# Routed experts: the first slot's expert chosen from the first 16 tiles, its weights loaded under the last dense group, and the gates gathered from memory

## The reference, cut to what matters

```python
def _moe2_ref(x, expert_emb, tau, w1, w2):        # N, D, E, F = 3072, 384, 8, 1024
    xn = x / (norm(x) + 1e-06)
    en = expert_emb / (norm(expert_emb) + 1e-06)
    logits = xn @ en.T / tau
    expert_idx = np.argmax(logits, axis=1)
    probs = np.exp(logits - logits.max(-1, keepdims=True))
    probs /= probs.sum(-1, keepdims=True) + 1e-09
    gate_w = probs[np.arange(N), expert_idx]
    for e in range(E):
        mask = expert_idx == e
        h = np.maximum(x[mask] @ w1[e], 0.0)
        out[mask] = gate_w[mask, None] * (h @ w2[e])
...
def reference(**kwargs):
    attn_out = _attn_ref(**attn_kwargs)            # B, H, S, D = 4, 8, 768, 48: delta rule
    x = attn_out.transpose(0, 2, 1, 3).reshape(B * S, H * D)
    x = _moe_ref(x=x, **moe_kwargs)                # all 8 experts on all rows, Sinkhorn gates
    return _moe2_ref(x=x, **moe2_kwargs)           # each row to its best expert
```

## Time and profile before

| | us |
|---|---|
| median of three runs | 2285.17 (2283.51 to 2286.48) |
| the profiled execution's own time | 2289.73 |
| its span, first to last instruction | 2287.9 |
| TensorE busy | 2201.0 (96%) |
| DVE busy | 1013.8 (44%) |
| ACT busy | 600.7 (26%) |
| POOL busy | 96.5 (4%) |

### The profile page before, as it was taken

One profiled execution on the slowest core, in us unless ns is written; L12 is line 12 of the kernel. 1 busy time (PEld: TensorE's weight loads), 2 busy tenths in 40 slices (PEclk: granted clock), 3 DMA queues, 4 the chain that ended last, 5 costly groups with the idle time before them and its releaser, 6 DMA issues.

```text
span 2287.9 us, 42621 instructions
## 1 busy us (share of the span) xinstructions
PE 2201.0 (96%) x17911; PEld 2041.4 (89%) x17911; DVE 1013.8 (44%) x1888; ACT 600.7 (26%) x1019; POOL 96.5 (4%) x91
## 2 busy tenths in 40 slices
PE   4899999999999999999999999999999998799998
PEld 4888899999999998999999899999999998699998
DVE  7676556245333333333233332323333235767774
ACT  2323222331111111111111111111111122366664
POOL 0000000000000000000000000000000000122221
PEclk7799999999999999999999999999999999699999
DMA  9545543340000000000000000000000011667662
GB/s 315 158 136 140 145 127 109 87 159 28 1 28 1 29 28 1 28 1 28 1 28 28 1 28 1 28 1 28 1 1 1 1 42 42 210 241 249 231 234 73
DMA packets 152504, 172.69 MB, mean 75 GB/s; under 512 B 81580, under 2 KB 112464, under 8 KB 152338
## 3 DMA queue, kind: packets, MB, share of 16 engines
q1 hardware_dynamic: 143090, 158.70, 21.6%
q0 software_dynamic: 3968, 10.82, 1.2%
q10 hardware_dynamic: 5280, 0.66, 0.2%
HBM read 144.19 MB, written 27.33 MB: 75 GB/s over the span
## 4 chain that ended last, share of the span: by engine, by line
PE 88%; DVE 5%; DMA 2%; SPq 2%; issue 2%; ACT 1%; POOL 0%; POOLq 0%; ACTq 0%; DVEq 0%
PE psA L1703 22%; PE psH L1720 16%; PE psB L1703 9%; PE psB L1720 8%; PE psY L1720 8%; PE psY L1845 6%; PE psH L1597 4%; PE psY L1612 3%; PE psB L1831 3%; PE psA L1831 3%; PE psA L1478 3%; DVE products L1046 1%; DVE sx L1049 1%; DMA r_scratch<-sr 1%; SPq L405 1%
## 5 line engine op out<-in xcount | busy, mean ns | idle before, releaser
L1703 PE MATMUL psA<-X,wh 128*128 128x512 f32 x1440 | 449.4, 393 | 1.8 <-DVE acc L1068 0.9
L1214 DVE SCALAR_TENSOR_TENSOR hl<-psA,hh 128x512 fp32r<-128x512 f32 x240 | 165.7, 690 | 626.6 <-ACT hh L846 626.5
L846 ACT ACTIVATE hh<-psA 128x512 fp32r<-128x512 f32 x240 | 143.3, 597 | 830.3 <-PE psA L1703 830.3
L1703 PEld LDWEIGHTS psA<-X,wh 128*128 128x128 f32 x1440 | 265.9, 188 | 47.5 <-issue 3.4
L1703 PE MATMUL psA<-X,wl 128*128 128x512 f32 x720 | 284.9, 396 | 0.0
L1720 PE MATMUL psH<-wh,hh 128*128 128x384 f32 x672 | 228.3, 340 | 0.0
L1720 PE MATMUL psH<-wh,hl 128*128 128x384 f32 x672 | 227.2, 338 | 0.0
L1720 PE MATMUL psH<-wl,hh 128*128 128x384 f32 x672 | 225.8, 336 | 0.0
L1214 DVE SCALAR_TENSOR_TENSOR hl<-psB,hh 128x512 fp32r<-128x512 f32 x96 | 66.3, 691 | 277.4 <-ACT hh L846 277.3
L1703 PE MATMUL psB<-X,wh 128*128 128x512 f32 x576 | 179.2, 392 | 0.0
L1438 DVE TENSOR_TENSOR vl<-vs,vh 128x768 fp32r<-128x768 f32 x152 | 145.6, 961 | 56.6 <-ACT vh L891 56.2
(11 more groups left out here) (282 smaller groups left out, 4122.9 us busy)
## 6 DMA issues: line engine op xcount, KB each, us to landing
vs<-v_d SPq DMA_DIRECT2D x38, 768.0 KB, 6.0
vs<-v_d SPq DMA_DIRECT2D x19, 1536.0 KB, 11.8
ws<-w_d SPq DMA_DIRECT2D x28, 768.0 KB, 6.0
kT<-kT_d SPq DMA_DIRECT2D x17, 512.0 KB, 5.3
qT<-qT_d SPq DMA_DIRECT2D x15, 512.0 KB, 5.3
a_scratch<-an SPq DMA_DIRECT2D x12, 512.0 KB, 4.0
kq<-kn_d SPq DMA_DIRECT2D x6, 768.0 KB, 6.2
vn<-vn_d SPq DMA_DIRECT2D x12, 384.0 KB, 4.9
```

What stands on the lines that cost most here:

```text
L846: act.activation(hh[kk % 3][:, :], ps_h[kk % (2 if last else 3)], ACT.Relu).then_inc(hh_ready, 1)
L1214: dve.scalar_tensor_tensor(hl[b][:, :], ps_h[bank], 0.0, hh[b][:, :].bitcast(F32), ALU.max, ALU.subtract).then_inc(hl_ready, 1)
L1703: mm = pe.matmul(to, a[half][:, c, col], X[:, 2 * g:2 * g + 2, b, c, :], start=(n == 0), stop=(n == 3 * KC - 1))
```

## The change

What it does, part by part:

1. `choose(0)`, `prefixes(0)`, `ranks(0)` and `places(0)` run one step earlier in the last expert, `counts(0)` on TensorE too. `places` 4 and 8 stand before `choose(1)`.
2. `most_rows` (five small DVE instructions) finds the expert with the most rows in tiles 0 to 15, `star`. `order_of_big` (five more) makes an order of experts in which it comes first, and `grown` uses it for the big slots; three instructions correct `eid` for it.
3. SP loads that expert's weights after the stores of the first ten chunks (groups 0 to 4), as soon as `star_i` and the first half's weight buffers are free. The buffers of the dense weights are laid out anew, so that slot 0's `vs` lie over the first half's, and the routing's small tensors over the dense hidden activations. Slot 1's weights now also wait for slot 0's rows (`xg_in[0]`).
4. ACT splits slot 0's eight pieces ahead of `features(0)`. DVE splits four ahead of it, two behind it and the last two in blocks 0 and 1 of slot 0. Slot 1's eight pieces are split two a block in blocks 4 to 7 of slot 0.
5. The gates' table, `entry_g` and its 24 products are gone. The norms and the exponential stand in blocks 1 and 2 of slot 0, the reciprocal in block 3. TensorE transposes the gates in block 4, DVE copies them, SP stores them to `g_dram` (two DMAs), and POOL gathers them by `who` for each slot (31 indirect DMAs of 128 values). ACT waits for them (`gates_in`) before it scales. TensorE's `features(1)` waits for DVE's copy.
6. `who` is written before the last instructions of `eid`.

```diff
-FIRST = 2
+FIRST = 4
+FIRST_LATE = 6
+GATED = 2
+SECOND_SPLIT = {4: (0, 1), 5: (2, 3), 6: (4, 5), 7: (6, 7)}
...
+                    if c == 2 * (NTA // GT + 1):
+                        sp.wait_ge(star_ready, 1)
+                        sp.wait_ge(l2_done, STEPS * (E - 2) + STEPS // 2)
+                        load_weights(sp.value_load(star_i[0:1, 0:1], min_val=0, max_val=E - 1), 0)
                     sp.wait_ge(acc_done, NALL - NT + GT * (c // 2 + 1))
...
                 sp.wait_ge(eid_ready, 1)
-                load_weights(0, 0)
-                load_weights(1, 1)
+                sp.wait_ge(xg_in[0], 16 * ST)
+                load_weights(expert_of(1), 1)
+                sp.wait_ge(gate_ready, 1)
+                for g in range(2):
+                    rows = g_dram[2 * g * S:2 * (g + 1) * S, :].rearrange("(t k) o -> t (k o)", k=C)
+                    sp.dma_start(rows, gate_rows[:, g * C:(g + 1) * C]).then_inc(gate_out, 16)
...
+                def gather_gates(i):
+                    for s in range(1 if SMALL[i] else ST):
+                        u = COLUMN[i] + s
+                        pool.indirect_dma_start(gates[:, u:u + 1], None, g_dram,
+                                                bass.IndirectOffsetOnAxis(who[:, u:u + 1], 0)).then_inc(gates_in[i % 2], 16)
...
                 gather(0)
                 gather(1)
+                pool.wait_ge(gate_out, 32)
+                gather_gates(0)
+                gather_gates(1)
                 for i in range(2, NSLOT):
                     gather(i)
                     scatter(i - 2)
+                    gather_gates(i)
...
-                        if last and kk == STEPS - 3:
+                        if last and kk == STEPS - 4:
                             choose(0)
-                        if last and kk == STEPS - 2:
+                        if last and kk == STEPS - 3:
                             prefixes(0)
-                        if last and kk == STEPS - 1:
+                        if last and kk == STEPS - 2:
+                            most_rows()
                             ranks(0)
+                        if last and kk == STEPS - 1:
+                            places(0)
+                            order_of_big()
...
-                        if next_small is not None:
+                        if not reached(i, 1):
+                            if f + FIRST_LATE < KF:
+                                split_piece(0, 0, f + FIRST_LATE)
+                            if f == GATED - 1:
+                                gate_norms()
+                            if f == GATED + 1:
+                                gate_values()
+                            if f == GATED + 2:
+                                gate_copy()
+                            for q in SECOND_SPLIT.get(f, ()):
+                                split_piece(1, 1, q)
+                        elif next_small is not None:
                             split_piece(i + 1, 1 - par, f)
...
-                    if kk == STEPS - 2:
+                    if kk == STEPS - 3:
                         counts(0)
...
+                        if f == GATED + 2 and not reached(i, 1):
+                            pe.wait_ge(gate_made, 1)
+                            pe.transpose(ps_gate, gate[:, :, :].rearrange("p b c -> p (b c)"), ident).then_inc(gate_turned, 1)
                         if f == 5 and after:
+                            if not reached(i, 1):
+                                pe.wait_ge(gate_ready, 1)
                             features(i + 1, 1 - par, *after)
...
                 features(0, 0, False, ST)
-                table(entry_g, entry_g_ready, ps_tab[1]).then_inc(tab_g_done, 1)
```

More of the change, by code:

```diff
@@ L160, in build @@
         w_at = top[0]
[L161 to L165, removed]
+        half_w = 4 * KC * FH
+        assert half_w == 4 * FB * DM
+        wh1, wh2, wl1, wl2 = [], [], [], []
+        for i in range(2):
+            wh1.append(keep(f"wh1_{i}", [P, KC, FH], F32R))
+            wh2.append(keep(f"wh2_{i}", [P, FB, DM], F32R))
+            wl1.append(keep(f"wl1_{i}", [P, KC, FH], F32R))
+            wl2.append(keep(f"wl2_{i}", [P, FB, DM], F32R))
         h_at = top[0]
@@ L175, in build @@
         kq = [keep(f"kq{i}", [P, 2 * NJ, D], at=at) for i, at in
[L176 to L179, removed]
+              enumerate([w_at, w_at + 4 * half_w, w_at + 5 * half_w, late_at, late_at + part, x_at + 4 * part])]
+        assert part == 4 * 2 * KC * SLOT == half_w
+        fh1 = [keep(f"fh1_{i}", [P, KC, FH], at=w_at + (4 * i + 2) * half_w) for i in range(2)]
+        fh2 = [keep(f"fh2_{i}", [P, FB, DM], at=w_at + (4 * i + 3) * half_w) for i in range(2)]
         hhA = [keep(f"hhA{i}", [P, SLOT], F32R, at=h_at + 4 * SLOT * i) for i in range(4)]
@@ L583, in _ @@
                 sp.wait_ge(rt_zero, 1)
[L584 to L592, removed]
-                    sp.dma_start(vs2[par][:, :, :], v2[bass.ds(which, 1)].rearrange("a (f p) d -> p (a f) d", p=P)).then_inc(vs_in[par][2], 16)
+                sp.dma_start(x2_dram[N:N + 1, :], zrow[0:1, :]).then_inc(zero_out, 16)
+                sp.dma_start(g_dram[N:N + 1, :], zrow[0:1, 0:1]).then_inc(zero_out, 16)
                 def refill(n, par):
@@ L1341, in _ @@
                 expert(E - 1, True)
-                places(0)
+                places(PLACED)
+                places(2 * PLACED)
                 choose(1)
-                places(PLACED)
+                places(3 * PLACED)
                 prefixes(1)
@@ L1427, in _, with gate_norms @@
[L1427 to L1430 removed]
+                def gate_norms():
+                    dve.wait_ge(rt_sqrt, 2)
+                    inverse_norm(nx[0][:, :], nx[1][:, :], nx[2][:, :])
+                    chain(rt, dve.tensor_tensor(lg[:, :, :], picked[:, :, :], rows_of(mxs[:, :]), ALU.subtract))
+                    dve.tensor_tensor(lg[:, :, :], lg[:, :, :], rows_of(nx[2][:, :]), ALU.mult).then_inc(lg_ready, 1)
@@ new lines, in gate_values, with gate_copy @@
+                def gate_values():
+                    dve.wait_ge(rt_exp, 1)
+                    chain(rt, dve.tensor_reduce(tilef[:, :], ex[:, :, :], AX.X, ALU.add))
+                    chain(rt, dve.tensor_scalar(rank[:, :], tilef[:, :], 1e-9, None, ALU.add))
+                    dve.reciprocal(gate[:, :, :].rearrange("p b c -> p c b"), rank[:, :].rearrange("p (c b) -> p c b", b=2)).then_inc(gate_made, 1)
+                def gate_copy():
+                    dve.wait_ge(gate_turned, 1)
+                    dve.tensor_copy(gate_rows[:, :], ps_gate).then_inc(gate_ready, 1)
@@ L1795, in _ @@
                 counts(1)
-                def table(what, ready, to):
-                    for t in range(NT):
-                        if t % PLACED == 0:
-                            pe.wait_ge(place_ready, t // PLACED + 1)
-                        if t % TABBED == 0:
-                            pe.wait_ge(ready, t // TABBED + 1)
-                        mm = pe.matmul(to, at_place[:, t, :], what[:, t, :, :].rearrange("p a b -> p (a b)"), start=(t == 0), stop=(t == NT - 1))
-                    return mm
-                table(entry, entry_ready, ps_tab[0]).then_inc(tab_done, 1)
+                for t in range(NT):
+                    if t % PLACED == 0:
+                        pe.wait_ge(place_ready, t // PLACED + 1)
+                    if t % TABBED == 0:
+                        pe.wait_ge(entry_ready, t // TABBED + 1)
+                    mm = pe.matmul(ps_tab, at_place[:, t, :], entry[:, t, :, :].rearrange("p a b -> p (a b)"), start=(t == 0), stop=(t == NT - 1))
+                mm.then_inc(tab_done, 1)
                 def features(i, par, small, loaded):
```

130 lines of the change are left out of this document (77 added, 53 removed).

## The result

The changed kernel is slower: 2299.85 us, median of five (2298.0 to 2308.28), against 2286.48 for the kernel before on the same chip (2283.51 to 2290.73); ratio 1.0061, 95% interval 1.0042 to 1.0079. The prediction was 2275.8 and faster. The profiled execution took 2298.32 us, its span is 2296.5, against 2289.73 and 2287.9 before.

The account below looks back on a forecast made before the run. TensorE was taken to bound the kernel, with only the hole between dense and routed stages able to pay. Seven terms summed to -9.4 us, from the median 2285.17 to 2275.8 us; range 2272.0 to 2281.5.

Parts of the forecast that it names:

- (1): Dense stage, first 16 tiles routed one step earlier: TensorE waits for DVE at the counts product, +1.1 us (+0.7 to +1.4).
- (2): Between the stages: the list of tokens `who` is done earlier, no longer behind the expert numbers, -1.75 us (-1.4 to -1.9).
- (3): First gather, with no weight loads beside it: lands in 3.0 us instead of 6.60, -3.6 us (0 to -4.5).
- (4): Before slot 0: without the gate table on TensorE the first hidden product follows `xgl` directly, -2.9 us.
- (5): Slot 0 without its hole: TensorE's 2.08 us wait and the clock fall behind it go, -3.95 us (bound -2.5).
- (6): Second half of slot 0: DVE splits slot 1's weights two pieces a step and falls slightly behind, +0.3 us (0 to +2).
- (7): Gates through memory: gathered gates come late, stalling slot 1's first give, counted from the first hidden product T, +1.4 us (0 to +3.5).
- rival C: Slot 1: gate gather lands like the slowest transfer, 14.9 us; stall 10.5, clock falls; +1.35, 2286.5 us; chance 0.04.
- signs of being wrong: Gather at 6 us, slot 0 over 20 us, or any wait over 4 us between the first and third slot.
- rival B: Slot 1: gates land at 7.9 us, stall 3.5, and the clock falls; -5.65, 2279.5 us; chance 0.13.

## Why the prediction was wrong

From one profiled execution of each kernel; all but the first term are counted from the second counts product on:

| term | predicted | measured |
|---|---|---|
| (1) wait at the counts product | +1.1 | +0.8 (TensorE idle 0.81 at 1907.00, released by DVE `oh`) |
| (2) list of tokens | -1.75 | -1.6 (17.6 to 16.1 from the counts product) |
| (3) first gather | -3.6 | -2.9 (it lands in 3.67, not 3.0) |
| (4) no gate table | -2.9 | -2.9 |
| (5), (6) slot 0 | -3.65 | -3.4 (22.46 to 19.09) |
| (7) gates late at slot 1's first give | +1.4 | +0.2 |
| the gate gathers' rows on POOL | 0 | +26.5 |
| POOL's drain at the end | 0 | +2.5 |

The traced execution of the changed kernel lost more in the loop than others do: the run with ACT's code moved has the same rows on POOL, shorter gaps in two of the five slots, and 355.7 us from the counts product to the end against 367.3. The price of the gathers by medians is the 17 to 20 us above.

**Terms 1 to 6 held**, each within its bounds where it had them, and the sum of the prediction, -9.4, is about what the kernel without gate DMAs gives: 2279.71 against 2287.93 for before on its chip, -8.2 (interval of the ratio -0.3 to -0.66%, 7 to 15 us). The loads of `vs` go out at 1916.12, 11 us earlier than I had put them by the clock of before; the dense stage there simply runs 10 us earlier in this execution. How long the attention stage takes differs between executions of programs in which it is the same (the first product behind it starts between 493.5 and 511.9 us in the runs shown), so a single span says little and the medians decide.

**Term 7 was right in kind and too large**: the gathers go out at T + 14.4 and TensorE waits 0.21 at the give. The landing was priced well: 5.8, and the run with the rows apart has a gate gather on its chain with 6.11 (from 1980.58), beside a median of 6.0 for the 128x384 gathers of the changed kernel. So 4-byte rows, whose slowness rival C rested on, land like the others. C asked how late a gate can come, and that was the wrong question. So were the signs of being wrong: the gather took 3.67, slot 0 19.1 and the longest wait up to slot 2 was 3.9 on ACT, so none of them (6, 20, over 4) came up. All looked at the hole, and most of the loss lies behind it.

**The step that failed** is the sentence behind it, "Behind slot 1 the gathers have a whole slot of room". They have: none is ever late. I priced the 31 added DMAs by when they land and by who waits for them, and nothing by what their issue does to the rest. The order of POOL's program should have made me ask: in a small slot the feature gather already stands 0.3 us behind two scatters, and the change puts two more DMAs between them. The other half of the error is in the first paragraph, "the dense and the routed stage are back-to-back matmuls that the change leaves alone, so only that hole can pay": only the hole could pay, but the routed stage could cost. There TensorE has little room between a hidden product and the give that needs it (a signal 2.2 us late became a wait of 1.5), and behind four of the five waits stands a fall of the clock that costs more than the wait: five waits of 1.5 us are 7.5 of the 20.6 us, the rest, 13.1, is half clock (1.2 GHz). That a short wait costs a clock fall I had read off slot 0 for rival B, and did not carry to the loop.

**Term for the drain.** Its cost goes by the number of indirect DMAs: 7.08 us with none added, 8.47 with 17, 9.28 and 9.29 with 27, 9.62 with 31, that is 82 ns each. No row of before showed it.

**Open.** That long rows of indirect DMAs on POOL bring the late signals is shown: added to the kernel before they bring them, and broken up in the changed kernel they take them away. How POOL's issues hold TensorE's signals was not settled. Not ACT's code, not the element size between 4 and 384 bytes, not the kind of DMA, not the waits on `gates_in`, and not full DMA engines alone (above). Some long rows leave no gap, and there POOL is the slow one: in the changed kernel's slot 15 (six in the row) two of its issues take 1.77 and 1.67 us instead of 0.98, in its slot 3 (five) 1.75 and 1.56. In the kernel before with extra gathers the same six in slot 15 have issues of 0.99 and 0.96, and the gap is there (2.61). So it may be that POOL and TensorE take turns at something. That was only seen, not tried. The 3.9 us gap in slot 1 of the changed kernel belongs to eleven DMAs with one pause of 0.66 us, and is gone without gate DMAs; in the version with the rows apart slot 1 still takes 0.9 more, which I did not follow up.

## What to carry to other kernels

A DMA that nobody waits for is not free: count what an issuing engine sends back to back before and after a change, and keep POOL's rows of indirect DMAs short (three here) by tying the optional ones to a later signal; a few lines turned 1.0061 into 0.9978. Where TensorE runs with less than a microsecond of room between a product and its use, price every new event beside it by the stall and by the clock fall behind it. Where an engine seems to wait for nothing, look at the releaser before forming a theory on the waiting engine: "<-PE psA" was right, and the ends of matmuls, which are modelled, had misled me.

## What the runs showed of the hardware

- A row of indirect DMAs on POOL, 0.30 us apart, can hold TensorE's semaphore signals until about its end: in the small slots the `gh` that waits for them has a gap of 0.5 us with three in the row, of 1.2 with four (ten times; once 0.5) and of 1.9 or 2.6 with five (once 1.3), and TensorE's matmuls are shown as going on meanwhile. Where two of POOL's own issues in such a row take 1.5 us or more (slots 3 and 15), there is no gap. 384-byte elements do it as 4-byte ones do. A pause of 1.6 us behind the third ends it.
- Each indirect DMA that the program has issued adds 0.082 us to POOL's drain at its end (7.08 us with 62, 9.62 with 93).
- Behind a wait of TensorE of 1.3 to 1.5 us the granted clock can fall to 1.2 GHz for some microseconds, in 14 of 19 cases: stretches of 14 to 18 us around the five waits of the changed kernel have a mean clock of 1.00, 0.89, 0.89, 0.79 and 0.81. Behind eight waits of 0.6 to 0.7 us it did not fall.
- Beside weight loads a gather of 128 elements of 4 bytes landed 6.1 us behind its issue, one of 128x384 in a median of 6.0.
